# The head of an attention, MoE and FFN kernel: w loaded as rows and turned, u loaded as one row and spread by a product with ones

## The chip, the cores and the metric

The kernel runs on one core of a Trainium2 chip. The metric is device time in microseconds of one execution; lower is better. Inputs and the output are float32 in DRAM.

## What is computed

Three stages follow each other. The first is a linear attention with decay, for 4 batches, 8 heads, 768 steps and head size 48; `w` (8 x 48) is the decay per head and channel, `u` (8 x 48) a factor for the current step:

```python
for t in range(S):
    kt, vt, rt = (k[:, :, t], v[:, :, t], r[:, :, t])
    cur = np.einsum('bhd,bhe->bhde', u[None] * kt, vt)
    y[:, :, t] = np.einsum('bhd,bhde->bhe', rt, state + cur)
    state = w[None, :, :, None] * state + np.einsum('bhd,bhe->bhde', kt, vt)
```

Its output, 3072 rows of 384, goes through a soft mixture of 8 experts (`phi`, `w1`, `w2`), and then through a feed-forward layer of width 2048 with an ELU (`w_in`, `w_out`).

## The kernel before

The attention works in 6 chunks of 128 steps; a unit is one chunk of one batch (24 units, `UNITS`). Inside a unit the decay is taken out by tables of powers of w: r is multiplied by w to the power of the step (`tables_T[:, 0]`), k by its inverse (`tables_T[:, 1]`), so that scores are one product of turned r and turned k. Heads stand in pairs, 64 partitions for each, of which 48 are used (`HP`, `D`). The five engines each run their own program, written out by hand, and meet in semaphores.

The head, up to the first scores, goes as follows.

- **SyncE** (`sync`) waits for GpSimd's first memset (`cleared`), loads w twice into `wcol`, transposed by the access pattern (`w_cols`, L428 to L431), one copy for each half of the partitions, then the first r (`load_r(0, 0)`, three DMAs from `load`, L375 to L377). Then it waits for the first k and loads k, r and v of batches 2 and 3, two pieces of w1, and goes on to the loop `load_chunk`, which refills k, r and v of each pair of batches when their readers are done.
- **ScalarE** (`scalar`) loads the first k (L375 to L377), does one Exp (L1292) that brings its table in, loads u into `u_row`, the same row for all 128 partitions (L1293), copies w into `wpow` (L1296, `w_copied`), issues four loads of phi (L1301), waits for the doubled table and copies its swapped half (L1304, `table_swapped`), loads the first v, and copies the turned table out of PSUM to `k_table` (L1307).
- **GpSimd** (`gpsimd`) sets constants (L488 to L519), waits for u and k, and forms r*u*k of units 0 and 1 in four products (L544, L547, twice); later it scales k (L527) and forms the same products for the following units (L535, L538).
- **VectorE** (`vector`) waits for w (`w_loaded`), takes its reciprocal (L996), and doubles the tables in six steps of two products (L1004 squares the powers, L1007 doubles the table), then L1014 twice, L1019 (which waits for `table_swapped`) and L1022. After it come r into `r_pair` (L1035), k into `k_pair` (L1080), the sum of r*u*k (`bonus`, L1028), k of unit 1 scaled into `k_nat` (L1084), and r and bonus of unit 1.
- **TensorE** (`tensor`) starts when `ones` is set with four products of ones (L598) whose results nobody reads, of 512, 512, 256 and 256 columns, then turns r of unit 0 (L603), k (L626), r of unit 1, and the table (L739); `keep_clock_up` (L593) adds products of ones; `attend` (L643) makes the scores. `turn_k(1, ...)` waits for L1084 (`k_scaled`), and then `key_values` (L667) needs the first v.

The loop after that repeats per unit: `key_values`, turns, state, values, scores. The expert and feed-forward stages follow; the diff does not touch them.

## Time and profile before

| | us |
|---|---|
| median of 3 runs | 393.62 |
| lowest and highest | 391.74, 393.88 |
| profiled execution | 392.18 |
| its span, first to last instruction | 390.4 |
| TensorE busy | 374.2 |
| VectorE, ScalarE, GpSimd busy | 267.6, 219.6, 103.3 |

The page gives busy time of each engine, then the span in 40 slices of 9.8 us (a digit is a tenth of a slice), then the chain that ended last. A timeline row gives the start, the duration, the engine, the line and what is written from what, and in brackets how long the engine stood idle before it and what ended that. ACTq and SPq rows are DMA issues: their duration is the issuing, not the transfer.

### The profile page before, as it was taken

The numbers are of one execution on the slowest core, as the hardware profiler recorded it, in microseconds if no ns is written. First come the engines' busy times: TensorE is split into PE (matmuls) and PEld (weight loads), VectorE is DVE, ScalarE is ACT, GpSimd is POOL, SyncE is SP. The second block draws the span as 40 slices with busy tenths as digits, with TensorE's granted clock in tenths as the row PEclk, the third lists the DMA queues.
The fourth block names the chain that finished last, engine by engine and source line by source line (L and its number), as shares of the span: only waits on it lengthen the run. The fifth ranks groups of instructions, "written<-read, shape, count | busy, mean of one in ns | idle before, by whom it ended". The sixth has DMA issues, their size and how long they took to land.

```text
span 390.4 us, 11439 instructions
## 1 busy us (share of the span) xinstructions
PE 374.2 (96%) x4373; PEld 333.0 (85%) x4373; DVE 267.6 (69%) x512; ACT 219.6 (56%) x498; POOL 103.3 (26%) x136
## 2 busy tenths in 40 slices
PE   6898999999889999999999999999999999999996
PEld 3787898989775454589999999999999999999996
DVE  4787788778767620699867767667777667776671
ACT  2896778777772131588564446444644464455441
POOL 7797777777640000355200000000000000000000
PEclk9999999999999999999999999999999999999999
DMA  7989899999999999920020002000200020002002
GB/s 152 254 151 186 199 234 233 227 255 254 235 303 426 430 432 403 373 64 2 0 83 1 2 0 81 0 0 0 81 0 0 0 81 0 0 0 82 2 2 81
DMA packets 87280, 51.80 MB, mean 133 GB/s; under 512 B 77776, under 2 KB 83024, under 8 KB 85200
## 3 DMA queue, kind: packets, MB, share of 16 engines
q1 hardware_dynamic: 82368, 50.21, 43.1%
q10 hardware_dynamic: 4880, 1.16, 1.4%
q8 instruction: 19, 0.31, 0.3%
q14 instruction: 13, 0.11, 0.1%
HBM read 45.86 MB, written 4.72 MB: 130 GB/s over the span
## 4 chain that ended last, share of the span: by engine, by line
PE 79%; DMA 10%; SPq 3%; issue 3%; ACT 3%; DVE 1%; POOL 1%; DVEq 0%; POOLq 0%; ACTq 0%
PE psum L976 17%; PE psum L978 17%; PE psum L977 17%; PE psum L911 6%; DMA w_out_raw<-in_moe_w_out_dram 4%; PE psum L603 4%; DMA r_raw<-in_r_dram 3%; PE psum L643 3%; PE psum L826 3%; PE psum L686 3%; PE psum L667 2%; PE psum L656 2%; PE psum L696 2%; DMA v_sb<-in_v_dram 1%; PE psum L703 1%
## 5 line engine op out<-in xcount | busy, mean ns | idle before, releaser
L978 PE MATMUL psum<-w_out_hi,elu_lo 128*128 128x384 f32 x372 | 125.8, 338 | 0.0
L976 PE MATMUL psum<-w_out_hi,elu_hi 128*128 128x384 f32 x372 | 125.7, 338 | 0.0
L977 PE MATMUL psum<-w_out_lo,elu_hi 128*128 128x384 f32 x372 | 125.3, 337 | 0.0
L1405 ACT ACTIVATE exp_h<-psum 128x512 f32<-128x512 f32 x96 | 57.6, 600 | 97.3 <-PE psum L911 97.0
L1246 DVE SCALAR_TENSOR_TENSOR elu<-psum,neg_part 128x512 f32<-128x512 f32 x96 | 66.3, 690 | 57.1 <-ACT neg_part L1392 57.1
L977 PEld LDWEIGHTS psum<-w_out_lo,elu_hi 128*128 128x128 f32 x372 | 69.8, 188 | 3.9
L976 PEld LDWEIGHTS psum<-w_out_hi,elu_hi 128*128 128x128 f32 x372 | 70.4, 189 | 0.0
L978 PEld LDWEIGHTS psum<-w_out_hi,elu_lo 128*128 128x128 f32 x372 | 69.9, 188 | 0.0
L1238 DVE TENSOR_TENSOR elu_lo<-elu,elu_hi 128x512 fp32r<-128x512 f32 x96 | 66.3, 691 | 0.6
L1280 ACT ACTIVATE scores<-ident_wide,bonus 128x128 f32<-128x128 f32 x192 | 58.8, 390 | 5.0 <-DVE bonus L1028 4.9
L1392 ACT ACTIVATE neg_part<-exp_h 128x512 f32<-128x512 f32 x96 | 60.0, 626 | 1.7 <-DVE elu L1246 1.3
L1259 DVE CAST elu_hi<-elu 128x512 fp32r<-128x512 f32 x96 | 44.0, 458 | 0.6
L1041 DVE COPY_PREDICATED scores<-mask,psum 128x512 f32<-128x512 uint32 x48 | 33.3, 736 | 15.3 <-PE psum L643 12.9
L911 PE MATMUL psum<-c_T,G_T 128*128 (+1 forms) x96 | 37.6, 397 | 0.8 <-DMA G_T<-G_parts 0.6
L686 PE MATMUL psum<-scores,v_sb 64*64 64x128 f32 (+1 forms) x768 | 25.9, 245 | 1.8 <-issue 1.6
L527 POOL TENSOR_TENSOR k_nat<-k_raw,k_table 128x384 f32<-128x384 f32 x23 | 23.2, 1009 | 15.6 <-PE psum L667 7.9
L584 POOL TENSOR_TENSOR w_out_lo<-w_out_raw,w_out_hi 128x384 fp32r<-128x384 f32 x16 | 16.8, 1058 | 34.4 <-ACT w_out_hi L1387 34.4
L686 PEld LDWEIGHTS psum<-scores,v_sb 64*64 64x64 f32 x768 | 22.4, 133 | 2.8 <-issue 2.8
L538 POOL TENSOR_TENSOR k_raw<-k_raw,r_raw 128x384 f32<-128x384 f32 x22 | 22.1, 1006 | 6.0 <-DMA r_raw<-in_r_dram 4.7
L643 PE MATMUL psum<-r_pair,k_pair 48*64 48x128 f32 (+1 forms) x768 | 20.9, 245 | 1.8 <-DVE r_pair L1035 1.8
L535 POOL TENSOR_TENSOR k_raw<-k_raw,u_row 128x384 f32<-128x384 f32 x22 | 22.1, 1006 | 1.7
L911 PEld LDWEIGHTS psum<-c_T,G_T 128*128 128x128 f32 x96 | 18.1, 190 | 3.5 <-issue 1.7
(155 smaller groups left out, 403.6 us busy)
## 6 DMA issues: line engine op xcount, KB each, us to landing
w<-in_moe_w_dram SPq DMA_DIRECT2D x8, 1536.0 KB, 13.6
w_sb<-in_moe_w_dram SPq DMA_DIRECT2D x8, 1024.0 KB, 6.3
out_dram<-out_sb SPq DMA_DIRECT2D x24, 192.0 KB, 1.9
w_sb<-in_moe_w_dram SPq DMA_DIRECT2D x8, 512.0 KB, 6.2
w_out_raw<-in_moe_w_out_dram SPq DMA_DIRECT2D x4, 768.0 KB, 15.7
r_raw<-in_r_dram SPq DMA_DIRECT2D x12, 192.0 KB, 3.2
r_raw<-in_r_dram SPq DMA_DIRECT2D x24, 96.0 KB, 3.4
w_in_sb<-in_moe_w_in_dram SPq DMA_DIRECT2D x1, 2304.0 KB, 19.4
```

The costliest lines, as they stand in the source:

```text
L686: m = pe.matmul(ps_y[e * HP:e * HP + HP, two, q * P + cols.start:q * P + P], v_sb[rows, q, b, 2 * e + two, :], scores[rows, i, h, cols], s ...
L911: pe.matmul(banks[4 + f % RING][:, :], G_T[:, f * P:(f + 1) * P], c_T[:, bass.ds(i * BANK, BANK)], start=True, stop=True).then_inc(ffn_don ...
L976: pe.matmul(acc, hi, w_out_hi[:, f, :], start=(f == 0), stop=False)
L977: pe.matmul(acc, hi, w_out_lo[:, f, :], start=False, stop=False)
L978: m = pe.matmul(acc, lo, w_out_hi[:, f, :], start=False, stop=(f == KF2 - 1))
L1041: dve.copy_predicated(scores[:, i, two::2, :].rearrange("p (n a) t -> p n a t", n=2), mask[:, :, :].bitcast(U32).unsqueeze(2).broadcast_to ...
L1238: dve.tensor_tensor(elu_lo[:, f % RING, :], elu[:, f % 2, :], elu_hi[:, f % RING, :].bitcast(F32), ALU.subtract).then_inc(lo_done, 1)
L1246: dve.scalar_tensor_tensor(out=elu[:, f % 2, :], in0=banks[4 + f % RING][:, :], scalar=0.0, in1=neg_part[:, f % 2, :], op0=ALU.max, op1=AL ...
L1259: dve.tensor_copy(elu_hi[:, f % RING, :], elu[:, f % 2, :]).then_inc(hi_done, 1)
L1280: m = act.activation(scores[:, i, h, :], ident if h < H // 2 else ident_swap, ACT.Copy, scale=bonus[:, i, h:h + 1])
L1392: act.activation(neg_part[:, f % 2, :], exp_h[:, f % 2, :], ACT.Relu, bias=1.0, scale=-1.0).then_inc(neg_ready, 1)
L1405: act.activation(exp_h[:, f % 2, :], banks[4 + f % RING][:, :], ACT.Exp).then_inc(exp_done, 1)
```

## The change

- w is loaded once, as 8 rows of twice 48 numbers, into a corner of `tables_T` (`w_nat`) that GpSimd fills with ones before. TensorE turns it twice, into two PSUM banks (`ps_w`); VectorE reads its reciprocals from one, ScalarE copies its powers from the other. Both now wait for `w_turned`.
- u is loaded as one row into partition 0 of `u_row`, by ScalarE ahead of k. TensorE multiplies it with a column of ones into PSUM (`u_spread`), and ScalarE copies the result over `u_row` (`u_ready`), for which GpSimd now waits. The table is turned into the bank of the second copy of w only after `w_copied` and `u_ready`.
- The first v is issued by SyncE right behind the first r, no longer by ScalarE.
- Two of the four products of ones stand ahead of the new turns, two behind.

```diff
--- before.py
+++ after.py
@@ -115,7 +115,6 @@
         state_sum = place("state_sum", [P, PAIRS, D], F32)
         bonus = place("bonus", [P, 2, H], F32)
         mask = place("mask", [P, 2, P], F32)
-        wcol = place("wcol", [P, H], F32)
         wpow = place("wpow", [P, 8, 2, PAIRS], F32)
         exp_warm = place("exp_warm", [P, 1], F32)
         ATT_END = cursor[0]
@@ -213,6 +212,9 @@
         ps_x = banks[7].rearrange("p (a t) -> p a t", a=PAIRS)
         ps_k_first = psum[:, 2:4, 0:PAIRS * HP].rearrange("p s (a t) -> p s a t", a=PAIRS)
         ps_tab = banks[4].rearrange("p (h d) -> p h d", h=H)
+
+        w_nat, u_nat = tables_T[0:H, 0, 0, :], u_row[0:1, :, :].rearrange("p h d -> p (h d)")
+        ps_w, ps_u = (banks[4][:, 0:H], banks[0][:, 0:H]), banks[1][:, 0:DM]
         ps_warm = banks[5][:, 0:P]
 
 
@@ -230,7 +232,10 @@
         v_loaded = [sem(f"v_loaded{g}") for g in range(2)]
         u_loaded = sem("u_loaded")
         w_loaded = sem("w_loaded")
+        w_turned = sem("w_turned")
         w_copied = sem("w_copied")
+        u_spread = sem("u_spread")
+        u_ready = sem("u_ready")
         phi_loaded = sem("phi_loaded")
         w1_loaded = sem("w1_loaded")
         w2_loaded = [sem(f"w2_loaded{e}") for e in range(E)]
@@ -327,7 +332,6 @@
             return x.rearrange("b (i rev) t d -> rev b t i d", rev=2)
 
         r_dram, k_dram, v_dram = by_sets(r), by_sets(k), by_sets(v)
-        w_cols = w.rearrange("h d -> d h")
         u_flat = u.rearrange("h d -> (h d)").rearrange("(o n) -> o n", o=1)
         phi_rows = phi.rearrange("(half two q d) s -> half two d q s", q=2, half=2, two=2)
         w1_dram = w1.rearrange("e (p c) f -> e p c f", p=P)
@@ -381,9 +385,10 @@
             return x_sb[:, UNITS - 2 + un, 0:DM].rearrange("p (rev i d) -> p rev i d", rev=2, d=D)
 
 
-        w_halves = [(slice(two * HP, two * HP + HP),
-                     wcol[two * HP:two * HP + HP, :].rearrange("p (e two rev) -> p two rev e", two=2, rev=2)[:, two])
-                    for two in range(2)]
+        w_halves, w_halves_too = (
+            [(slice(two * HP, two * HP + HP),
+              turned[two * HP:two * HP + HP, :].rearrange("p (e two rev) -> p two rev e", two=2, rev=2)[:, two])
+             for two in range(2)] for turned in ps_w)
 
         block = ctx.enter_context(nc.Block())
 
@@ -426,10 +431,9 @@
                         load_w1(range(2, E), slice(2, KD))
 
             sp.wait_ge(cleared, 1)
-            for half in range(2):
-                sp.dma_start(wcol[half * HP:half * HP + D, :], w_cols, allow_slow_non_contiguous=True
-                             ).then_inc(w_loaded, 16)
+            sp.dma_start(w_nat.rearrange("h (two d) -> h two d", two=2)[:, :, 0:D], w.unsqueeze(1).broadcast_to([H, 2, D])).then_inc(w_loaded, 16)
             load_r(0, 0)
+            load_v(0, 0)
             sp.wait_ge(k_loaded[0], LOADED)
             load_k(0, 1)
             load_r(0, 1)
@@ -485,7 +489,7 @@
 
         @block.gpsimd
         def _(pool):
-            pool.memset(wcol[:, :], 1.0).then_inc(cleared, 1)
+            pool.memset(w_nat, 1.0).then_inc(cleared, 1)
             pool.memset(v_sb[:, :, :, :, D:HP], 0.0).then_inc(cleared, 1)
             pool.memset(phi_sb[:, :, :], 0.0).then_inc(cleared, 1)
             pool.memset(ones[:, :], 1.0).then_inc(ones_set, 1)
@@ -538,7 +542,7 @@
                 pool.tensor_tensor(k_raw[:, :, b], k_raw[:, :, b], r_raw[:, :, b, :, 0:D], ALU.mult).then_inc(ruk_done, 1)
 
 
-            pool.wait_ge(u_loaded, 16)
+            pool.wait_ge(u_ready, 1)
             pool.wait_ge(k_loaded[0], LOADED)
             for un in range(2):
                 pool.tensor_tensor(ruk_first(un), k_raw[:, :, un], u_sets, ALU.mult).then_inc(ru_done, 1)
@@ -594,9 +598,21 @@
 
 
             pe.wait_ge(ones_set, 1)
-            for i, n in ((2, 4), (3, 4), (6, 2), (5, 2)):
+            def fill(i, n):
                 pe.matmul(banks[i][:, 0:n * P].rearrange("p (n t) -> p n t", n=n), ones[:, :],
                           ones[:, :].unsqueeze(1).broadcast_to([P, n, P]), start=True, stop=True)
+
+            fill(2, 4)
+            fill(6, 2)
+
+            pe.wait_ge(const_set, 5)
+            pe.wait_ge(w_loaded, 16)
+            for at in ps_w:
+                pe.transpose(at, w_nat, ident[0:H, 0:H]).then_inc(w_turned, 1)
+            pe.wait_ge(u_loaded, 16)
+            pe.matmul(ps_u, ones[0:1, :], u_nat, start=True, stop=True).then_inc(u_spread, 1)
+            fill(3, 4)
+            fill(5, 2)
 
             def turn(turned, nat, last_pairs):
                 for a in range(PAIRS):
@@ -728,13 +744,14 @@
                 return m
 
 
-            pe.wait_ge(const_set, 5)
+            pe.wait_ge(w_copied, 1)
             pe.wait_ge(pads_set, 1)
             turn_r(0, 0, 0)
             pe.wait_ge(k_loaded[0], LOADED)
             turn_k_first()
             turn(banks[7], r_pair_raw(1), ident_swap).then_inc(r_turned, 1)
             pe.wait_ge(tables_done, 3)
+            pe.wait_ge(u_ready, 1)
             for a in range(PAIRS):
                 m = pe.transpose(banks[4][:, a * P:(a + 1) * P], tables_T[:, 1, a, :], ident[:, :])
             m.then_inc(table_turned, 1)
@@ -990,7 +1007,7 @@
 
 
 
-            dve.wait_ge(w_loaded, 32)
+            dve.wait_ge(w_turned, 2)
             dve.memset(tables_T[:, 0, :, HP:HP + 1], 1.0).then_inc(powers, 1)
             for rows, cols in w_halves:
                 m = dve.reciprocal(wpow[rows, 0, 1, :].rearrange("p (rev e) -> p rev e", rev=2), cols)
@@ -1287,14 +1304,16 @@
                          ps_y[:, :, 0:2 * P].rearrange("p two (q t) -> p two q t", q=2)).then_inc(yT_ready, 1)
 
 
+            act.dma_start(u_nat, u_flat).then_inc(u_loaded, 16)
             load(act, k_raw, k_dram, 0, 0, k_loaded)
             act.wait_ge(const_set, 5)
             act.activation(exp_warm[:, :], ident[:, 0:1], ACT.Exp)
-            act.dma_start(u_row[:, :, :].rearrange("p h d -> p (h d)"), u_flat.broadcast_to([P, DM])).then_inc(u_loaded, 16)
-            act.wait_ge(w_loaded, 32)
-            for rows, cols in w_halves:
+            act.wait_ge(w_turned, 2)
+            for rows, cols in w_halves_too:
                 m = act.copy(wpow[rows, 0, 0, :].rearrange("p (rev e) -> p rev e", rev=2), cols)
             m.then_inc(w_copied, 1)
+            act.wait_ge(u_spread, 1)
+            act.copy(u_row[:, :, :].rearrange("p h d -> p (h d)"), ps_u).then_inc(u_ready, 1)
             act.wait_ge(cleared, 3)
             for half in range(2):
                 for two in range(2):
@@ -1302,7 +1321,6 @@
                                   ).then_inc(phi_loaded, 16)
             act.wait_ge(powers, 15)
             act.copy(tables_T[:, 1, 2:PAIRS, 0:HP], tables_T[:, 1, 2:PAIRS, HP:P]).then_inc(table_swapped, 1)
-            load(act, v_sb, v_dram, 0, 0, v_loaded)
             act.wait_ge(table_turned, 1)
             act.copy(k_table[:, :, :], ps_tab[:, :, 0:D]).then_inc(table_ready, 1)
             diagonals(0, 0, 0)
```

TensorE at the start of its program, before (names: `ident_wide` is the identity; L598 are the products of ones, L603 turns, L626 turns of k, L739 the turned table):

```order
L598 MATMUL psum<-ones 128x512 [waits ones_set]
L598 MATMUL psum<-ones 128x512
L598 MATMUL psum<-ones 128x256 x2
L603 MATMUL psum<-ident_wide,r_raw 128x128 [waits r_loaded0,pads_set,const_set]
L603 MATMUL psum<-ident_wide,r_raw 128x128 x3
L626 MATMUL psum<-ident_wide,k_raw 48x64 [waits k_loaded0]
L626 MATMUL psum<-ident_wide,k_raw 48x64 x15
L603 MATMUL psum<-ident_wide,r_raw 128x128 x4
L739 MATMUL psum<-ident_wide,tables_T 128x128 [waits tables_done]
L739 MATMUL psum<-ident_wide,tables_T 128x128 x3
```

and in the changed kernel (L602 products of ones, L611 the turns of w, L613 the product for u, L619 turns, L642 turns of k, L756 the turned table):

```order
L602 MATMUL psum<-ones 128x512 [waits ones_set]
L602 MATMUL psum<-ones 128x256
L611 MATMUL psum<-ident_wide,tables_T 128x8 [waits w_loaded,const_set]
L611 MATMUL psum<-ident_wide,tables_T 128x8
L613 MATMUL psum<-u_row,ones 128x384 [waits u_loaded]
L602 MATMUL psum<-ones 128x512
L602 MATMUL psum<-ones 128x256
L619 MATMUL psum<-ident_wide,r_raw 128x128 [waits r_loaded0,pads_set,w_copied]
L619 MATMUL psum<-ident_wide,r_raw 128x128 x3
L642 MATMUL psum<-ident_wide,k_raw 48x64 [waits k_loaded0]
L642 MATMUL psum<-ident_wide,k_raw 48x64 x15
L619 MATMUL psum<-ident_wide,r_raw 128x128 x4
L756 MATMUL psum<-ident_wide,tables_T 128x128 [waits u_ready,tables_done]
L756 MATMUL psum<-ident_wide,tables_T 128x128 x3
```

Between the products of ones now stand three products that wait for the loads of w and u, and the table's turn waits for `u_ready` besides.

ScalarE from its table load to the copy of the turned table, before:

```order
L1292 ACTIVATE exp_warm<-ident_wide 128x1 [waits const_set]
L1293 DMA u_row<-in_u_dram 128x384
L1296 COPY wpow<-wcol 64x4 [waits w_loaded]
L1296 COPY wpow<-wcol 64x4
L1301 DMA phi_sb<-in_moe_phi_dram 48x2x32 [waits cleared]
L1301 DMA phi_sb<-in_moe_phi_dram 48x2x32 x3
L1304 COPY tables_T<-tables_T 128x2x64 [waits powers]
L375 DMA v_sb<-in_v_dram 128x8x48
L376 DMA v_sb<-in_v_dram 64x8x48
L377 DMA v_sb<-in_v_dram 64x8x48
L1307 COPY k_table<-psum 128x384 [waits table_turned]
```

and in the changed kernel, where the issue of u (L1307) stands ahead of the three of k:

```order
L1310 ACTIVATE exp_warm<-ident_wide 128x1 [waits const_set]
L1313 COPY wpow<-psum 64x4 [waits w_turned]
L1313 COPY wpow<-psum 64x4
L1316 COPY u_row<-psum 128x384 [waits u_spread]
L1320 DMA phi_sb<-in_moe_phi_dram 48x2x32 [waits cleared]
L1320 DMA phi_sb<-in_moe_phi_dram 48x2x32 x3
L1323 COPY tables_T<-tables_T 128x2x64 [waits powers]
L1325 COPY k_table<-psum 128x384 [waits table_turned]
```

The issues of phi (`phi_sb`) stand behind the copy of u out of PSUM, the copy inside `tables_T` comes behind them as before, and the three issues of v are gone.

## Rows read from the trace of the kernel before

**Rows 1.** The page: busy time of TensorE, and the DMA share in 40 slices.
```profile
PE 374.2 (96%) x4373; PEld 333.0 (85%) x4373; DVE 267.6 (69%) x512; ACT 219.6 (56%) x498; POOL 103.3 (26%) x136
...
DMA  7989899999999999920020002000200020002002
```

**Rows 2.** The chain of waits, head (start us, us, what).
```profile
3.34 4.47 DMA r_raw<-in_r_dram
...
12.20 0.63 PE psum L603 x4
...
13.94 0.52 PE psum L667 x16
...
14.62 1.00 POOL k_nat L527
```

**Rows 3.** Timeline, ScalarE (start, us, engine, line, op, out<-in, [idle before <-releaser]).
```profile
0.82 0.47 ACTq L375 DMA_DIRECT2D k_raw<-in_k_dram  x1
...
4.49 0.20 ACT L1296 COPY wpow<-wcol 64x4 f32<-64x4 f32 x1 [0.21 <-DMA wcol<-in_w_dram]
...
4.87 1.42 ACTq L1301 DMA_DIRECT2D phi_sb<-in_moe_phi_dram  x3
6.78 0.30 ACT L1304 COPY tables_T<-tables_T 128x128 f32<-128x128 f32 x1 [1.89 <-DVE tables_T L1007]
6.79 0.43 ACTq L375 DMA_DIRECT2D v_sb<-in_v_dram  x1
...
10.23 0.48 ACT L1307 COPY k_table<-psum 128x384 f32<-128x384 f32 x1 [3.15 <-PE psum L739]
```

**Rows 4.** Timeline, VectorE.
```profile
6.32 0.43 DVE L1007 TENSOR_TENSOR tables_T<-tables_T,wpow 128x256 f32<-128x256 f32 x1
...
7.33 0.28 DVE L1019 TENSOR_TENSOR tables_T<-tables_T,wpow 128x128 f32<-128x128 f32 x1
...
8.68 0.69 DVE L1035 TENSOR_TENSOR r_pair<-psum,tables_T 128x512 f32<-128x512 f32 x1 [1.00 <-PE psum L603]
...
10.74 1.36 DVE L1084 TENSOR_TENSOR k_nat<-k_raw,k_table 128x384 f32<-128x384 f32 x1 [0.28 <-ACT k_table L1307]
```

**Rows 5.** Timeline, GpSimd.
```profile
7.55 1.00 POOL L544 TENSOR_TENSOR x_sb<-k_raw,u_row 128x384 f32<-128x384 f32 x1 [1.46 <-DMA u_row<-in_u_dram]
...
10.67 1.01 POOL L547 TENSOR_TENSOR x_sb<-x_sb,r_raw 128x384 f32<-128x384 f32 x1
```

**Rows 6.** Timeline, GpSimd and VectorE in chunk 1.
```profile
31.47 1.01 POOL L538 TENSOR_TENSOR k_raw<-k_raw,r_raw 128x384 f32<-128x384 f32 x1 [0.17 <-DMA r_raw<-in_r_dram]
31.54 1.01 DVE L1057 COPY logits_T<-logits_now 128x128 f32<-128x128 f32 x1
```

**Rows 7.** Timeline, TensorE, head (PEld is a weight load).
```profile
1.72 4.50 PE L598 MATMUL psum<-ones 128*128 128x512 f32 x8 [1.72 <-POOL ones L491]
2.74 0.34 PEld L598 LDWEIGHTS psum<-ones 128*128 128x128 f32 x1 [0.52 <-issue]
...
3.59 0.34 PEld L598 LDWEIGHTS psum<-ones 128*128 128x128 f32 x1 [0.52 <-issue]
...
5.19 0.62 PEld L598 LDWEIGHTS psum<-ones 128*128 128x128 f32 x3 [0.41 <-issue]
...
7.95 0.63 PE L603 MATMUL psum<-ident_wide,r_raw 128*128 128x128 f32 x4 [1.73 <-DMA r_raw<-in_r_dram]
```

**Rows 8.** Stretch 4 to 6 us (last: clock, DMA share, GB/s); v loads; SyncE issues.
```profile
4.00:6.00 2.00, 2.00 (x6) 0.91 (x4) 1.45 (x14) 0.66 (x4) 1.53 (x7) 1.00 1.23 262
...
DMA to landing us min/median/max: 3.3/4.1/5.3
...
6.12 0.39 SPq L375 DMA_DIRECT2D k_raw<-in_k_dram  x1
...
14.82 0.38 SPq L375 DMA_DIRECT2D k_raw<-in_k_dram  x1
...
17.17 2.90 SPq L375 DMA_DIRECT2D r_raw<-in_r_dram  x1
```

## The prediction

> **What bounds the kernel now.** I read the page first: TensorE is busy 96% of the span and the DMA engines are near full for the first half [rows 1]. The diff touches only the head, so what counts is when TensorE gets into its steady row of work, and whether a later stage passes a shift on. The chain of waits shows the head [rows 2]: the last piece of the first r lands 4.47 us after 3.34, at 7.81; TensorE turns r at 7.95 [rows 7], needs the scaled k of unit 1 at 12.20 and multiplies k and v from 13.94; GpSimd scales the k of unit 2 at 14.62. From there on the chain is TensorE, with waits on loads that consumers release. I take 14.6 us as the hand-over point: what the change has won or lost there I carry to the end.
>
> The profiled execution took 392.18 us around its span of 390.4; the median of the three runs is 393.62, which is 1.4 higher. My shift is worked out in the profiled execution and added to the median.
>
> **Loads.** w was 2 DMAs with a packet for every number, now one of 16 rows; SyncE saves one issue of about 0.5, so r is issued from 1.4 instead of 2.02. u was 192 KB (one row to 128 partitions), now 1.5 KB; its issue, some 0.45, now stands ahead of k's, which moves from 0.82 to 1.3 [rows 3]. Both feed the same engines, which move 262 GB/s in the stretch from 4 to 6 us [rows 8]: k and r are 768 KB, 2.9 us of that rate. Starting near 2.5 they are in by about 6.0 to 6.3. k was in at 6.1 (SyncE, which waits for it, goes on at 6.12) [rows 8], so k gains nothing, r about 1.6. The first v (3 issues) goes into SyncE's gap from 3.96 to 6.12, where they fit; it used to leave ScalarE at 6.79 to 8.80 [rows 3] and land 3.3 to 5.3 after issue [rows 8], by some 13.4, under TensorE's warm-up products that end at 13.94. I cost that move at nothing; without that cover its gain would count.
>
> **TensorE's head.** A warm-up product of 512 columns is two passes of 0.85 (2.74 to 3.59); from 5.19 on three weight loads, one per pass of 256 columns, take 0.62 together, so a pass is some 0.2, half the time per column [rows 7]. So the clock was at 1.2 GHz until about 5.1 and at 2.4 after it, with unbroken work from 1.72 on. (The granted clock is printed as 1.00 in the stretch from 4 to 6 us, so the steps tell more here than that column.) Now fills of 512 and 256 columns end at 1.72 + 1.71 + 0.85 = 4.28. The two turns of w: four warm turns of 128 columns take 0.63 [rows 7], so at most 0.3 each at half clock and at least a bare load and 8 columns, 0.15: w is turned at 4.6 to 4.9; I take 4.8. The product for u, 384 columns in two passes, is 0.64 at 2.4 GHz and 1.28 at 1.2 (from the same steps); begun cold and ended warm it is done at about 5.65. ScalarE copies 128x384 out of PSUM in 0.48 [rows 3]: u is ready at 6.2, instead of 7.5. Fills of 512 and 256 columns follow, 1.28 warm: 5.6 to 6.95. So r is turned from 6.95, 1.0 earlier than 7.95; the fills, not r, end last.
>
> **ScalarE.** The table load and exp ended at 4.28 (0.21 idle before 4.49); they move 0.5 later, still about when w is turned. But the four phi issues, 1.8 us (0.34 + 1.42 and gaps), used to start at 4.50 and now stand behind the copy of u: 6.2 to 8.0. Queued behind them is the copy that swaps the table (0.30, formerly 6.78) [rows 3]. VectorE's last table step waits for it, so its next step, r into r_pair, cannot start before 8.0 + 0.30 + 0.28 + 0.15 + gaps = 8.8; it was 8.68 [rows 4]. Thus r_pair gains nothing at all even though r comes 1.6 earlier. The turned table does gain, since TensorE reaches it sooner: at 8.7 to 9.35. ScalarE copied it to k_table from 10.23 to 10.71; now it can at 9.4 to 9.9 [rows 3].
>
> **VectorE against GpSimd, the term that decides.** GpSimd was free at 6.09 and waited 1.46 for u before its four products of 1.0 each [rows 5]. They began at 7.55, when the table chain was practically over (7.61). Now k and u are there at 6.2, so the four products start near 6.3, while VectorE, 0.4 later than before (4.8 plus the copies of w), still has 1.4 us of table products ahead. What happens then is seen once in this head: L1084, a product of two SBUF operands, 128x384, started at 10.74 beside GpSimd's L547 (10.67 to 11.68) and took 1.36 [rows 4, 5]. By the 128 and 256 column products (0.28, 0.43) it should take 0.57; it ended 0.42 after GpSimd's product did. The copy L1057 at 31.54 took 1.01 beside L538, and ended with it too [rows 6]. So a VectorE instruction of this kind stands until GpSimd's is over. In the Trainium skill, SBUF — State Buffer, Who interferes with whom, says that a VectorE instruction with two SBUF inputs contends with a GpSimd instruction that reads SBUF, and that whoever issued second blocks fully. By that rule the sum comes to +0.2 to +1.3 (below), and to the first rival's -0.95 without it; L1084 agrees.
>
> All remaining table products are of that kind, and they hang on each other. Bounds: one block (GpSimd takes the first turn and VectorE's row then runs through) puts r_pair at about 9.15; four blocks in turn put it at about 11.0. I take two, the middle of what the gaps between dependent products allow: VectorE stands from 6.4 to 7.3, works to 8.05, stands to 9.05, and the last table step ends near 9.9. Then r_pair 9.95 (was 8.68), k_pair until 11.3, the reduction (0.54) until 11.85, k_nat (0.57) until 12.45, instead of 12.10. Sum at 12.2: r and the turned table earlier, but **+0.35 us** net (one block +0.2, since k_nat then meets GpSimd's fourth product; four blocks k_nat ends at 13.4, +1.3; and -0.1 if k_nat finds GpSimd idle).
>
> **Does the shift last?** The copy of k_nat is followed by the turn, five fills and key_values, as before. SyncE's issues are slowed by full queues (the r load at 17.17 took 2.90) [rows 8]. With 190 KB and some 770 tiny packets gone its row runs about 1 us ahead, so no load becomes the new end. Later loads are released by consumers, the weights of the experts too, so they shift along. 393.62 + 0.35 is about **393.9 us**. A difference under 0.5%, 2.0 us, is about what a measurement of this kernel cannot tell from none.
>
> **Rivals.**
> 1. *No block, or one that fits in.* If the products run side by side, r_pair is at 8.8, k_pair ends at 10.2, the reduction at 10.65, and k_nat, alone, at 11.15: -0.95, so 392.7. For it: the table step at 7.33 still ran when GpSimd began at 7.55 and took its 0.28 [rows 4, 5], though there VectorE was first. Against it: L1084. Chance 0.25.
> 2. *The clock stays low.* TensorE's unbroken row is cut at 4.3 by the tiny turns and the wait for u. If it stays at 1.2 GHz past 5.1, the u product takes 1.28 and the fills 2.56, r is turned at 8.8 (+0.85). If it stays there until 12.2, the turns and products between 7.95 and 10.2 (2.25 us) take twice that, less what VectorE's lateness hides: up to +1.9 more, 2.7 in all, 396.3. This is the slower side; it passes 0.5% only if the clock is still low through most of the turns up to about 11 us. For it: before, the clock rose after an unbroken row. Against: once up it stayed up through the idle 1.73 ahead of 7.95 [rows 7]: the four turns behind it took 0.63. Chance 0.13.
> 3. *The load stream was the bound.* If the attention stage runs on SyncE's row, what counts is when k of the next chunk is issued: 14.82 before [rows 8], at best 12.9 with unslowed issues; -1.9, 391.7. Against: TensorE waits for loads only briefly before 36 us. Chance 0.12.
> 4. The forecast, two blocks or its neighbours: 0.50.
>
> **Numbers.** From 391.7 (rival 3) to 396.0 (the clock for most of the head) and the spread of 2 us between runs: 391.5 to 396.0. Faster by over 0.5%: most of rival 3 and a little of rival 1, 0.13. Slower: rival 2's upper part and four blocks that grow later, 0.15. Between: 0.72.
>
> **What would show it.** In the changed profile: GpSimd's first product near 6.3; a table product of about 1 us beside it; r_pair's first step after 9; k_nat's end at 12.3 to 13.4; weight loads of 0.19 from about 5.2 on. The steps are wrong if all table products keep their 0.16 to 0.43 (rival 1), if the fills before r show 0.34 weight loads (rival 2), or if the span falls by more than what is won at 14.6 us (rival 3). If u is ready after 7.5, the collision term falls.

## The result, and the profile after

| | before | changed |
|---|---|---|
| median of 20 runs each, us | 393.71 | 394.82 |
| lowest and highest | 391.56, 395.65 | 391.8, 398.3 |
| ratio, 95% interval | | 1.0054 [1.0032, 1.0076] |
| profiled execution, its span | 392.18, 390.4 | 394.29, 392.6 |

The ratio leaves out two executions of the changed kernel, 398.14 and 398.3, that lie over 1.5% above its fastest. By it the change costs 0.5%, about 2.1 us, just over the bound up to which the prediction spoke of no change; the two medians of the table differ by less, 1.11 us or 0.28%. So the cost is clear of zero, but its size is known only as 0.3% to 0.8%. The forecast of 393.9 is 0.9 below the measured median. What was forecast as +0.35 us at the end of the head came out as +2.0 there.

The page of the changed kernel, lines of its parts 1 and 4:

```profile
PE 377.5 (96%) x4377; PEld 334.4 (85%) x4377; DVE 269.2 (69%) x512; ACT 220.5 (56%) x499; POOL 104.6 (27%) x136
...
PE 81%; DVE 5%; DMA 4%; issue 3%; SPq 3%; ACT 1%; POOL 1%; POOLq 0%; DVEq 0%
```

TensorE has 3.3 us more [rows 1]: a share of that is the product for u and products of ones at half clock. VectorE, which held 1% of the chain before and nothing of its first 17 us, holds 5% of it, 18.9 us, of which 8.5 lie in the first 17 us. The rest lies behind the head, and the split differs between single executions (16.7 and 3.7 in the second profile). The chain of waits of the changed kernel, head (start, us, what):

```profile
7.43 0.87 DVE wpow L1021
...
8.67 1.51 DVE tables_T L1031 x2
...
10.91 0.95 DVE wpow L1039
...
11.89 0.69 DVE r_pair L1052
```

Before, the chain up to 12.20 was the load of r and TensorE's turns [rows 2]; now it is the table of powers on VectorE. The timeline shows why. GpSimd and VectorE (L1021, L1024, L1031 and L1039 are table products, as L1036 is, L548 and L551 GpSimd's products of r, u and k, L521 and L523 GpSimd's memsets; a VectorE row's start can lie a little before the end of the one ahead of it):

```profile
5.10 0.17 DVE L1013 RECIPROCAL wpow<-psum 64x4 f32<-64x4 f32 x1 [5.10 <-issue]
5.36 0.31 POOL L521 MEMSET k_nat<- 128x256 f32 x1
5.50 0.69 DVE L1016 COPY tables_T<-wpow 128x4 f32<-128x4 f32 x1
...
5.86 0.31 POOL L523 MEMSET state<- 128x256 f32 x1
6.23 0.17 DVE L1024 TENSOR_TENSOR tables_T<-tables_T,wpow 128x8 f32<-128x8 f32 x1
...
7.01 0.16 DVE L1021 TENSOR_TENSOR wpow<-wpow 128x8 f32<-128x8 f32 x1
7.13 1.15 POOL L548 TENSOR_TENSOR x_sb<-k_raw,u_row 128x384 f32<-128x384 f32 x1 [0.97 <-ACT u_row L1316]
7.34 0.96 DVE L1021 TENSOR_TENSOR wpow<-wpow 128x8 f32<-128x8 f32 x1
8.36 1.14 POOL L551 TENSOR_TENSOR x_sb<-x_sb,r_raw 128x384 f32<-128x384 f32 x1
8.67 2.12 DVE L1031 TENSOR_TENSOR tables_T<-tables_T,wpow 128x256 f32<-128x256 f32 x2
9.46 1.18 POOL L548 TENSOR_TENSOR x_sb<-k_raw,u_row 128x384 f32<-128x384 f32 x1
...
10.71 1.13 POOL L551 TENSOR_TENSOR x_sb<-x_sb,r_raw 128x384 f32<-128x384 f32 x1
10.91 0.95 DVE L1039 TENSOR_TENSOR wpow<-wpow 128x4 f32<-128x4 f32 x1
...
13.56 0.55 DVE L1101 TENSOR_TENSOR k_nat<-k_raw,k_table 128x384 f32<-128x384 f32 x1
```

Each of GpSimd's four products has one VectorE product that stands until it is over: L1021 ends at 8.30 and GpSimd's first at 8.28; L1039 ends at 11.86 and the fourth at 11.84. L1021 works on 8 columns and took 0.16 when nothing stood beside it, as at 7.01. The groups by shape (busy us, mean ns) part the two L1031, the second and third block, and L1039:

```profile
L1031 DVE TENSOR_TENSOR tables_T<-tables_T,wpow 128x256 f32<-128x256 f32 x1 | 1.1, 1107 | 0.0
L1031 DVE TENSOR_TENSOR tables_T<-tables_T,wpow 128x128 f32<-128x128 f32 x1 | 1.1, 1085 | 0.0
L1039 DVE TENSOR_TENSOR wpow<-wpow 128x4 f32<-128x4 f32 x1 | 1.0, 954 | 0.0
```

GpSimd pays too: 1.13 to 1.18 us a product where it took 1.00 [rows 5].

SyncE, ScalarE and TensorE of the changed kernel in the same stretch:

```profile
6.58 0.38 SPq L379 DMA_DIRECT2D k_raw<-in_k_dram  x1
...
6.57 0.48 ACT L1316 COPY u_row<-psum 128x384 f32<-128x384 f32 x1 [1.16 <-PE psum L613]
6.58 2.46 ACTq L1320 DMA_DIRECT2D phi_sb<-in_moe_phi_dram  x4
9.08 0.30 ACT L1323 COPY tables_T<-tables_T 128x128 f32<-128x128 f32 x1 [2.04 <-DVE tables_T L1024]
...
4.91 1.62 PE L613 MATMUL psum<-u_row,ones 1*128 1x384 f32 x2
6.46 2.93 PE L602 MATMUL psum<-ones 128*128 128x512 f32 x4
7.48 0.34 PEld L602 LDWEIGHTS psum<-ones 128*128 128x128 f32 x1 [0.52 <-issue]
9.19 0.94 PE L619 MATMUL psum<-ident_wide,r_raw 128*128 128x128 f32 x4
```

k is in at 6.57 (SyncE goes on at 6.58; 6.12 before [rows 8]). The product for u ends at 6.53 and the fills (the products of ones) start at 6.46 with weight loads of 0.34, the step of half clock [rows 7]. r is turned from 9.19 instead of 7.95.

**The sum, now from measured rows.** The reciprocals start 0.60 later (5.10; 4.50 before). The copy L1016, 0.69 for an operation that takes 0.17 elsewhere, puts the chain back by another 0.54: the first doubling L1024 starts at 6.23, and at 5.09 before, so 1.14 in all. The four blocks cost 0.80 + 0.68 + 0.80 + 0.80 = 3.08. From the old end of the table, 7.68, that gives 11.90, and the row ends at 11.86. VectorE used to stand idle 1.00 there [rows 4], so r_pair starts 3.21 later (11.89). Of this 1.19 comes back by k_nat: with GpSimd finished, k_nat takes 0.55 instead of 1.36, there is no wait of 0.28 for k_table, and the rest is 0.10 of gaps. k_nat ends at 14.11 instead of 12.09: **+2.02 us**.

### The profile page after: what moved, and what is told of

The parts are those of the page before. It is cut to its first block, busy times and chain, and to the rows that moved or that the text cites. A ratio compares the mean times of both kernels' runs of the same rounds, so it can differ in the third digit from the quotient of the medians.

```text
span 392.6 us, 11449 instructions
## 1 busy us (share of the span) xinstructions
PE 377.5 (96%) x4377; PEld 334.4 (85%) x4377; DVE 269.2 (69%) x512; ACT 220.5 (56%) x499; POOL 104.6 (27%) x136
## 4 chain that ended last, share of the span: by engine, by line
PE 81%; DVE 5%; DMA 4%; issue 3%; SPq 3%; ACT 1%; POOL 1%; POOLq 0%; DVEq 0%
PE psum L993 17%; PE psum L994 17%; PE psum L995 17%; PE psum L928 6%; DMA r_raw<-in_r_dram 4%; PE psum L619 3%; PE psum L659 3%; PE psum L702 3%; PE psum L863 3%; PE psum L843 3%; PE psum L712 2%; PE psum L672 2%; PE psum L683 2%; SPq L380 1%; SPq L379 1%
## 5 line engine op out<-in xcount | busy, mean ns | idle before, releaser
L659 PEld LDWEIGHTS psum<-r_pair,k_pair 48*64 48x64 f32 x768 | 18.9, 133 | 4.9 <-issue 4.6
```

The lines of the kernel that those rows point to most:

```text
L659: m = pe.matmul(ps_A[two][e0:e0 + HP, a, cols], k_pair[rows, i, a, e0:e0 + HP], r_pair[rows, i, a, cols], start=True, stop=True, skip_grou ...
```

## Experiments

All runs compute the whole of the reference; none leaves a part out. Each was compared with the kernel before in runs on the same chip. Three chips were used, so kernels are set against each other by their ratios and not by their medians. "k_nat" is the end of its first product, the head's last step: 12.09 before, 14.11 changed. Times of steps come from the one profiled execution of each kernel.

### GpSimd's products wait for the table

```diff
             pool.wait_ge(u_ready, 1)
+            pool.wait_ge(tables_done, 3)
+            pool.wait_ge(powers, DECAY_SET)
             pool.wait_ge(k_loaded[0], LOADED)
```

> The changed kernel, but GpSimd starts its four products of k, u and r only when VectorE's table chain is through (tables_done 3 and the last power). Theory A (the collision of these products with the table products is the main loss): table products keep 0.16 to 0.43 us, r_pair starts near 10.2 instead of 11.89 (then TensorE's late turn of r ends last), k_nat ends near 13.2 instead of 14.11, and the first scores start 1 us or more earlier than 13.29; the time falls by about 1 us against the changed kernel. Theory B (the low clock of TensorE is the main loss): r_pair at 10.2 too, but k_nat and the first scores move by less than 0.4 us, time unchanged within 0.3 us.

Measured: 394.48 of 12 runs, ratio 1.0014 [0.9979, 1.0049]. The rows that the collision had stretched:

```profile
7.36 0.16 DVE L1023 TENSOR_TENSOR wpow<-wpow 128x8 f32<-128x8 f32 x1
...
7.94 0.63 DVE L1033 TENSOR_TENSOR tables_T<-tables_T,wpow 128x256 f32<-128x256 f32 x2
9.43 0.29 DVE L1038 TENSOR_TENSOR tables_T<-tables_T,wpow 128x128 f32<-128x128 f32 x1 [0.86 <-ACT tables_T L1325]
9.64 0.15 DVE L1041 TENSOR_TENSOR wpow<-wpow 128x4 f32<-128x4 f32 x1
10.04 1.00 POOL L550 TENSOR_TENSOR x_sb<-k_raw,u_row 128x384 f32<-128x384 f32 x1 [3.85 <-DVE wpow L1041]
10.36 0.69 DVE L1054 TENSOR_TENSOR r_pair<-psum,tables_T 128x512 f32<-128x512 f32 x1 [0.56 <-PE psum L621]
12.67 0.82 DVE L1103 TENSOR_TENSOR k_nat<-k_raw,k_table 128x384 f32<-128x384 f32 x1
```

With the four products away, every table product has its own duration again, and the table is ready at 9.79 instead of 11.86. So the blocks are shown: the same instructions, less only what stood beside them. The first scores start at 12.50 (13.29 changed), 0.8 earlier where the expectation wanted 1 or more. The time moved from 1.0054 to 1.0014, but the two intervals overlap, so the gain is seen in the head and not shown in the time. And k_nat gains just 0.62 (13.49), because two things that the blocks had covered now show: the swap stands behind the phi issues (0.86 idle), and r's turn ends last (0.56 idle); and the delayed GpSimd products meet the reduction and k_nat instead.

### The product for u behind all products of ones; and both edits together

```diff
-            pe.wait_ge(u_loaded, 16)
-            pe.matmul(ps_u, ones[0:1, :], u_nat, start=True, stop=True).then_inc(u_spread, 1)
             fill(3, 4)
             fill(5, 2)
+            pe.wait_ge(u_loaded, 16)
+            pe.matmul(ps_u, ones[0:1, :], u_nat, start=True, stop=True).then_inc(u_spread, 1)
```

> The changed kernel, but TensorE's product for u stands behind all four products of ones, so only the two tiny turns of w interrupt them. Theory A: the clock does not matter much; the collision stays (u is ready near 7.5, the products start near 7.6 and still meet three table products), k_nat ends at 13.5 or later. Theory B: the record of the clock starts at 5 to 6 us instead of 9.86, r is turned from about 7.3, and k_nat ends 1 us or more earlier. If the clock record still starts after 8 us, the two turns of w alone are enough to hold the clock low.

> Both edits together: products of GpSimd behind the table chain, product for u behind the products of ones. If A and B each hold a part, r_pair starts near 9.6 (bound by phi issues and the swapped copy on ScalarE), k_nat ends near 12.3 as in the kernel before, and the time is within 0.3% of the kernel before. If neither is the cause, the time stays at 1.005 of before.

Measured: alone 397.43 of 11 runs, 1.0083 [1.005, 1.0116]; with GpSimd's wait 395.73 of 12, 1.0054 [1.0023, 1.0084]. The first is the slowest kernel of the study. ScalarE of the first of them:

```profile
8.82 0.48 ACT L1316 COPY u_row<-psum 128x384 f32<-128x384 f32 x1 [3.40 <-PE psum L615]
8.83 1.92 ACTq L1320 DMA_DIRECT2D phi_sb<-in_moe_phi_dram  x4
10.79 0.30 ACT L1323 COPY tables_T<-tables_T 128x128 f32<-128x128 f32 x1 [1.49 <-issue]
```

Of the first expectation only "k_nat ends at 13.5 or later" came true (14.73), with u ready at 9.30 and not at 7.5; the second wanted k_nat near 12.3 and the time within 0.3% of before, and neither came. The clock did rise earlier, at 7.94 and 7.17 by the trace's record (9.86 changed), and r was turned from 8.71 and 8.38 (9.19). The copy of u waits 3.40, the four phi issues wait behind it in ScalarE's program, and the swap behind those; the table ends at 12.48 and, in the combination, at 11.14. In the first one whole block is left (L1039, 0.96 from 11.53) and a short one (L1036, 0.48), in the second none, and the queue on ScalarE has taken their place. In the combination k_nat ends latest of all (14.83), since the reduction waits for GpSimd products that begin at 11.38. So these two runs show what a late u costs on ScalarE; they don't weigh the blocks against the clock.

### v issued by SyncE, alone

```diff
             load_r(0, 0)
+            load_v(0, 0)
...
-            load(act, v_sb, v_dram, 0, 0, v_loaded)
```

> The kernel before with the one edit that SyncE issues the first v right behind the first r. The prediction costed it at nothing: first scores at 10.6 us, key_values at 13.9, ratio to before within 0.998 to 1.002. Rival: v ahead in the queue delays k (it stood between k, w and r) and the loads of batches 2 and 3, so the first k lands after 6.5, GpSimd is unaffected (it waits for u till 7.5), and the time rises by 0.3 to 1 us.

Measured (kernel before with this move): 394.65 of 12 runs, 1.0007 [0.9974, 1.0041]; k_nat 12.26, +0.17, which is what the kernel before shows in its own second profile (12.27). Costed at nothing in the prediction, and it is nothing that these runs can tell.

### The two halves of the change

The changed kernel with u loaded to 128 partitions as before (w and v changed):

```diff
-            pool.wait_ge(u_ready, 1)
+            pool.wait_ge(u_loaded, 16)
...
-            pe.wait_ge(u_loaded, 16)
-            pe.matmul(ps_u, ones[0:1, :], u_nat, start=True, stop=True).then_inc(u_spread, 1)
...
-            pe.wait_ge(u_ready, 1)
...
-            act.dma_start(u_nat, u_flat).then_inc(u_loaded, 16)
...
+            act.dma_start(u_row[:, :, :].rearrange("p h d -> p (h d)"), u_flat.broadcast_to([P, DM])).then_inc(u_loaded, 16)
...
-            act.wait_ge(u_spread, 1)
-            act.copy(u_row[:, :, :].rearrange("p h d -> p (h d)"), ps_u).then_inc(u_ready, 1)
```

> The changed kernel with u loaded as before (one DMA of 192 KB to 128 partitions, issued by ScalarE behind its Exp) and no product for u. Theory A (collision): u lands at about 7.5 as before, so GpSimd's products start near 7.6 while the table chain, which starts at 5.1, ends near 8.4 undisturbed: two or three table products still meet them, r_pair near 10 to 10.5, k_nat's end at 12.8 to 13.4. Rival (the early start of the table chain's own inputs matters, not GpSimd): the table chain starts at 5.1, 0.6 after before, and k_nat's end is 0.6 late, 12.7, with no table product over 0.6 us except the copy of the reciprocal (0.7, beside memsets).

And the kernel before with the u part alone (the same lines the other way round, the product between the fills of 512 and 256 and of 512 and 256 columns):

> The kernel before with only u changed: one row, product with ones, copy out of PSUM, GpSimd waits for that. Theory A: the table chain starts at 4.5 and would end at 7.6; u is ready near 6.8, k near 6.3, so GpSimd starts near 6.9 and meets two table products; the phi issues stand behind the copy of u and end near 8.9, so the swapped copy comes at 8.9 instead of 6.8; r_pair near 9.6 to 10.5, k_nat's end 12.8 to 13.3. Rival: u earlier is harmless or good, r_pair at 8.7 to 9.0, k_nat's end at 12.1 or before.

Measured: w and v 394.01 of 12, 1.0020 [0.9981, 1.0058], k_nat 12.87, +0.78; u alone 393.55 of 12, 1.0026 [0.9991, 1.0061], k_nat 13.22, +1.13. The shifts add up to 1.91 against 2.02 for the whole, the ratios to 0.46% against 0.54%. Neither half alone can be told from no change in time. Both halves collide:

w and v, where u lands by its own load and only the table is late (two blocks; the second is on L1036, 0.96 from 9.48):

```profile
7.92 1.43 DVE L1028 TENSOR_TENSOR tables_T<-tables_T,wpow 128x256 f32<-128x256 f32 x2
8.19 1.02 POOL L548 TENSOR_TENSOR x_sb<-k_raw,u_row 128x384 f32<-128x384 f32 x1 [2.01 <-DMA u_row<-in_u_dram]
```

u alone, where GpSimd starts 0.66 earlier, and the table's first doubling waits 0.39 for ScalarE's copy of w (three blocks):

```profile
6.89 0.99 POOL L547 TENSOR_TENSOR x_sb<-k_raw,u_row 128x384 f32<-128x384 f32 x1 [0.79 <-ACT u_row L1305]
7.02 2.14 DVE L1020 TENSOR_TENSOR tables_T<-tables_T,wpow 128x256 f32<-128x256 f32 x2
8.88 1.06 PE L609 MATMUL psum<-ident_wide,r_raw 128*128 128x128 f32 x4
9.09 1.08 DVE L1025 TENSOR_TENSOR tables_T<-tables_T,wpow 128x128 f32<-128x128 f32 x1
```

### Also the swap ahead of the phi issues

```diff
+            act.wait_ge(powers, 15)
+            act.copy(tables_T[:, 1, 2:PAIRS, 0:HP], tables_T[:, 1, 2:PAIRS, HP:P]).then_inc(table_swapped, 1)
             act.wait_ge(cleared, 3)
...
-            act.wait_ge(powers, 15)
-            act.copy(tables_T[:, 1, 2:PAIRS, 0:HP], tables_T[:, 1, 2:PAIRS, HP:P]).then_inc(table_swapped, 1)
```

This, and GpSimd's wait of the first experiment.

> The changed kernel, GpSimd's products behind the table chain as in e1_products_wait, and ScalarE's four phi issues behind the copy that swaps the table. If the phi issues were the next limit: the last table product ends near 8.7 instead of 9.79, GpSimd starts near 8.9 instead of 10.04, and k_nat's end comes 0.6 to 1.0 before the 13.49 of e1. If TensorE's late turn of r (9.2 with the clock low) is the limit instead, r_pair stays at 10.2 to 10.4 and only GpSimd moves, k_nat's end within 0.4 of 13.49.

Measured: 394.41 of 12, 1.0051 [1.0013, 1.0089]. The table is done at 8.82, 3.0 earlier than in the changed kernel, and r_pair still starts at 10.36:

```profile
9.19 1.06 PE L621 MATMUL psum<-ident_wide,r_raw 128*128 128x128 f32 x4
10.36 0.69 DVE L1054 TENSOR_TENSOR r_pair<-psum,tables_T 128x512 f32<-128x512 f32 x1 [1.54 <-PE psum L621]
12.55 1.05 DVE L1103 TENSOR_TENSOR k_nat<-k_raw,k_table 128x384 f32<-128x384 f32 x1 [0.27 <-ACT k_table L1327]
```

VectorE now idles 1.54 for r's turn, which the fills at half clock hold until 9.19. k_nat ends at 13.60, no better than 13.49. k_nat itself takes 1.05 instead of 0.55, beside GpSimd's fourth product. The second bound under the blocks is TensorE.

### Rearranged: w turned once, one product of ones fewer, no collision

```diff
-            fill(6, 2)
...
-            for at in ps_w:
+            for at in ps_w[:1]:
                 pe.transpose(at, w_nat, ident[0:H, 0:H]).then_inc(w_turned, 1)
...
-            fill(5, 2)
+            fill(6, 2)
...
-            dve.wait_ge(w_turned, 2)
+            dve.wait_ge(w_turned, 1)
+            for rows, cols in w_halves:
+                m = dve.tensor_copy(wpow[rows, 0, 0, :].rearrange("p (rev e) -> p rev e", rev=2), cols)
+            m.then_inc(w_copied, 1)
...
+                if un == 1:
+                    pool.wait_ge(k_scaled, 1)
```

Besides these, the two edits of the last experiment; GpSimd's fourth product now waits for k_nat (`k_scaled`), and ScalarE's copies of w are gone.

> A try for a version that beats both: w is turned once, behind the first product of ones (near 3.6), VectorE copies w itself, one product of ones of 256 columns less, swapped copy ahead of the phi issues, GpSimd's products behind the table chain and its last one behind k_nat. The table chain starts near 4.1 and ends near 7.5; r lands at 7.2, is turned from 7.3 to 8.0; r_pair near 8.4, k_nat alone near 10.7 to 11.3 (12.09 before); the ratio to before 0.997 to 1.000. If it is not below 1.000 although k_nat's end is early, the head's gain is lost behind it (k of unit 0 scaled by GpSimd).

Measured: 393.01 of 12 runs, 1.0004 [0.9972, 1.0035]; k_nat 12.49. w is turned behind one fill only, the copy into the table starts before GpSimd's memsets and takes 0.17, the table ends at 7.86, and r_pair waits 1.54 for r's turn until 9.39. The time can't be told from that of before.

### w so, and u as before

```diff
             load_r(0, 0)
-            load_v(0, 0)
...
-            pool.wait_ge(u_ready, 1)
+            pool.wait_ge(u_loaded, 16)
...
+            load(act, v_sb, v_dram, 0, 0, v_loaded)
```

The w part as in the last kernel, with all four products of ones, three of them behind the turn of w; u (its load by ScalarE to all 128 partitions) and v as before; GpSimd's products no longer wait for the table, only the fourth waits, for k_nat.

> A second try for a version that beats both: the kernel before with w as rows, turned once behind the first product of ones and copied by VectorE; u and v loaded as before; GpSimd's last product behind k_nat. Table chain from near 4.2 to near 7.4, GpSimd from 7.5 (u's landing) so it meets nothing, clock up by 5 to 8 us, r turned at 7.7 to 8.0, k_nat undisturbed and ended at 11.1 to 11.4 (12.09 before). Ratio to before 0.997 to 1.000, which five rounds can hardly tell from 1.

Measured: 394.73 of 13 runs, 1.0025 [0.9987, 1.0063]. In the head it is the best kernel of all: k_nat ends at 10.92, 1.17 earlier than before, as k_nat stands beside no GpSimd product and takes 0.55. That GpSimd would meet nothing did not hold: its first product starts at 7.45, and L1037, a table product of 128 columns, takes 1.09 beside it instead of 0.28. The time doesn't show the gain. The rows show where it goes in this one execution (it took 401.88, 7 above the median, and the trace's clock drops at 47 and at 122 us, so its later part is not read):

```profile
7.51 1.09 DVE L1037 TENSOR_TENSOR tables_T<-tables_T,wpow 128x128 f32<-128x128 f32 x1
...
13.35 0.56 PE L682 MATMUL psum<-v_sb,k_nat 128*48 128x48 f32 x16 [0.58 <-DMA v_sb<-in_v_dram]
...
19.70 0.43 PE L701 MATMUL psum<-scores,v_sb 64*64 64x128 f32 x8 [1.60 <-issue]
```

The first v, again issued late by ScalarE, is what key_values waits for; half of the gain is gone there (13.35, and 13.87 before), and an idle stretch of 1.60 on TensorE for which no releaser is shown takes the rest. Whether v moved to SyncE would keep the gain wasn't tried, and with one execution profiled, and an unusually long one, it stays open whether the idle stretch belongs to the kernel: where the gain goes in the others is not shown.

### The product for u first of all

```diff
-            fill(2, 4)
...
+            pe.wait_ge(u_loaded, 16)
+            pe.matmul(ps_u, ones[0:1, :], u_nat, start=True, stop=True).then_inc(u_spread, 1)
             pe.wait_ge(const_set, 5)
             pe.wait_ge(w_loaded, 16)
...
-            pe.wait_ge(u_loaded, 16)
-            pe.matmul(ps_u, ones[0:1, :], u_nat, start=True, stop=True).then_inc(u_spread, 1)
+            fill(2, 4)
             fill(3, 4)
             fill(6, 2)
```

The rearranged kernel with nothing ahead of the product for u and the turn of w.

> As e8_rearranged, but TensorE's product for u is its first instruction, w's turn the second, and the products of ones follow without a break. Clock theory (a product of one row, 1.6 us at the low clock, inside the row of products of ones delays the clock): the record of the full clock starts at 6 to 8 us instead of 10.37, r is turned near 7.7 and k_nat ends near 11.7 instead of 12.49. Rival (the record's start is chance, 5 to 11 us in any kernel): it starts anywhere, also after 9.

Measured: 392.64 of 12 runs, 0.9987 [0.9948, 1.0025]. It loads w, u and v as the change does, and its interval lies below that of the changed kernel (whose lower end is 1.0032), though the two were not run against each other; from before it can't be told. VectorE and TensorE:

```profile
4.83 0.17 DVE L1021 COPY tables_T<-wpow 128x4 f32<-128x4 f32 x1
...
3.80 4.63 PE L606 MATMUL psum<-ones 128*128 128x512 f32 x6
8.22 1.06 PE L621 MATMUL psum<-ident_wide,r_raw 128*128 128x128 f32 x4
9.39 0.69 DVE L1057 TENSOR_TENSOR r_pair<-psum,tables_T 128x512 f32<-128x512 f32 x1 [1.73 <-PE psum L621]
```

The table is done at 7.66, and k_nat ends at 12.10, as before the change. What failed is the expectation on the clock: the row of fills from 3.80 on is unbroken and all at half clock (each pass of 512 columns 0.85 as in [rows 7]), and r's turn takes 1.06 instead of 0.63; VectorE idles 1.73 for it.

### Each kernel once more

> The changed kernel once more, for a second profile. The collision theory expects at least three table instructions of 0.9 us or more again and r_pair after 11; the clock theory expects the full clock from after 9 us again (9.86 in the first profile). If either is chance, it differs here.

> The kernel before once more, for a second profile. No table instruction over 0.5 us, GpSimd's first product at 7.5 to 7.7, r_pair at 8.7 to 9.0, k_nat's end near 12.1; full clock from 5 to 8 us (5.08 in the first profile, 7.53 in e4_v_by_sync_alone whose TensorE row is the same).

Measured: changed 395.02, span 393.3; before 393.35, span 391.6. Of the changed kernel the blocked rows return to within 0.02 us:

```profile
7.33 0.96 DVE L1021 TENSOR_TENSOR wpow<-wpow 128x8 f32<-128x8 f32 x1
8.66 2.12 DVE L1031 TENSOR_TENSOR tables_T<-tables_T,wpow 128x256 f32<-128x256 f32 x2
```

k_nat ends at 14.10; in the second look at before, at 12.27. What did move in before is the clock: the trace's record of its full level starts at 5.08 in the first look and at 7.47 in the second.

### All runs on one line

If a shift of the head went through to the end undiminished, a ratio should be the shift of k_nat over 393.7:

| kernel | k_nat ends | shift | as a ratio | measured, interval |
|---|---|---|---|---|
| u first, rearranged | 12.10 | +0.01 | 1.0000 | 0.9987 [0.9948, 1.0025] |
| v by SyncE alone | 12.26 | +0.17 | 1.0004 | 1.0007 [0.9974, 1.0041] |
| rearranged | 12.49 | +0.40 | 1.0010 | 1.0004 [0.9972, 1.0035] |
| w and v | 12.87 | +0.78 | 1.0020 | 1.0020 [0.9981, 1.0058] |
| u alone | 13.22 | +1.13 | 1.0029 | 1.0026 [0.9991, 1.0061] |
| products wait | 13.49 | +1.40 | 1.0036 | 1.0014 [0.9979, 1.0049] |
| and swap first | 13.60 | +1.51 | 1.0038 | 1.0051 [1.0013, 1.0089] |
| changed | 14.11 | +2.02 | 1.0051 | 1.0054 [1.0032, 1.0076] |
| u product last | 14.73 | +2.64 | 1.0067 | 1.0083 [1.005, 1.0116] |
| both | 14.83 | +2.74 | 1.0070 | 1.0054 [1.0023, 1.0084] |
| w early, u as before | 10.92 | -1.17 | 0.9970 | 1.0025 [0.9987, 1.0063] |

All but the last lie in their intervals, and the four kernels with the largest shifts, the changed one among them, are the four whose intervals lie wholly above 1. So a shift to the later side fits with passing on in full. More is not shown: the intervals are about as wide as the shifts, seven of the eleven hold 1.0000 as well, and the kernel before differs by 0.18 in k_nat's end between its own two profiles. The one clear gain did not show in the time.

## Why the prediction was right, and where it was not

- **The number.** The measured 394.82 lies between 391.5 and 396.0, and by the ratio the change is just over the 0.5% that parted "between" (0.72) from "slower" (0.15). That it lies in the range is in part luck: at the end of the head the prediction allowed its own mechanism +0.2 to +1.3, and +2.02 came. The upper end of the range was set for another reason, a clock low through most of the head (whose own worst case was 396.3).
- **The collision.** The mechanism, VectorE's table products standing behind GpSimd's, is shown by the first experiment. What was mis-sized is "I take two": four blocks came, in turn with GpSimd's four products. The section Who interferes with whom of SBUF — State Buffer in the Trainium skill says that the instruction issued second blocks fully; this trace agrees, with L1021 held for 0.96 where it takes 0.16, and ended 0.02 after GpSimd's. GpSimd's products are slowed as well, by 0.13 to 0.18. Because the table products hang on each other, one is always waiting when GpSimd's product ends, and GpSimd's next one is issued while VectorE's runs.
- **Even the four-block bound was short.** It said 13.4 for k_nat's end and 11.0 for r_pair; they were 14.11 and 11.89. Missing were 0.54 for the copy L1016 beside the memsets, which no sentence of the prediction had, and w turned later than "4.6 to 4.9": the first fills did not end at 4.28, the turns only start at 4.68 and are read at 5.10. GpSimd began at 7.13 and not near 6.3: u's product, two passes of 0.8 at half clock and so 1.62 where even the low-clock price was 1.28, ended at 6.53, and the copy out of PSUM at 7.05; k had come at 6.57. It began later, and still found four products of the table ahead of it, because the table was later as well.
- **The loads.** "r about 1.6" was 0.6: its last piece landed at 7.22 and at 7.81 before, and not at 6.0 to 6.3. It cost nothing in the changed kernel, where the fills hold TensorE until 9.19.
- **phi behind u.** "6.2 to 8.0" was 6.58 to 9.04: four issues of 2.46 in all, where before they took 0.34 + 1.42. In the changed kernel the blocks hide it; the products-wait kernel shows it as 0.86 idle.
- **TensorE's head, and rival 2.** "r is turned from 6.95" was 9.19, and the rise of the clock at 5.1 did not come: the fills still load weights in 0.34. The rival was right about the clock and had a chance of 0.13; it said 8.8, where its own terms, 4.8 + 1.28 + 2.56, give 8.64. It did not set the time: r_pair waited for the table until 11.89, while r's turn was done at about 10.1. It is the next bound, and in the kernels without the blocks it is the one that is seen (1.54 and 1.73 idle).
- **Rival 1**, no block, fell: its -0.95 needed table products of 0.16 to 0.43 beside GpSimd. **Rival 3**, the load stream, fell too: SyncE reached its w1 issue earlier (12.38, and 13.60 before), but the next k, which its readers release, went out at 15.32 and not 14.82 [rows 8], and the scores came 2.0 later. That issues are slowed "by full queues" is an inference; the rows show only how long they take.
- **The shift lasts.** Right as far as these runs can tell. Scores of the third and fourth unit are 2.0 later; the last of 24 starts 1.0 later in the one profile and 1.6 in the second (against their own look at before), the expert stage 3.2 and 2.9, the span 2.2 and 1.7 longer. The kernel before alone differs by 1.1 at the expert stage between its two profiles. In between single executions differ by idle stretches of TensorE without a shown releaser (1.48 at 114.83 and 1.00 at 121.77 in the changed kernel), so the table above over many runs is the better evidence.

## What to carry to other kernels

When a load is made faster, look at what its reader does once it is released: here GpSimd's four products were free as long as they came after the table, and cost 3.1 us of the table's chain when released into it. Of a chain of small dependent VectorE products like this one, count a block for every GpSimd product that can be issued beside it (four of four here, three with u alone, two with w and v), and keep the two apart by order. And before removing a bound, write down the next two under it: here ScalarE's issues and TensorE's clock stood right behind the blocks, so that taking the blocks away gave back 0.6 of 2.0 us.

## What the runs showed of the hardware that was not expected

**A copy beside memsets.** L1016 copies 4 columns and took 0.69 in the changed kernel, from 5.50 to 6.19, beside three memsets of GpSimd, the last of which ends at 6.17; it took 0.17 where it stood ahead of them (4.83 in the u-first kernel). L1021, issued behind it at 5.59, ends with it. Table products of up to 32 columns took 0.16 to 0.19 beside the same memsets in the kernel before, as they do elsewhere, so it is the copy and not any VectorE instruction. That the memsets hold it is read from these ends and not tested by moving them.

**A row of ones and the clock.** Start of the full clock (2.4 GHz; the lower level is 1.2) in the trace's record, by where the product of one row stands on TensorE (in one kernel, w and v, no usable value; there weight loads are down to 0.19 from 5.54 on):

| product of one row (K = 1) | starts of full clock, us |
|---|---|
| none in the head: before twice, v by SyncE, w early | 5.08, 7.47, 7.53, 6.23 |
| behind all fills: alone, and with GpSimd's wait | 7.94, 7.17 |
| ahead of or within the fills: changed twice, products wait, u alone, swap first, rearranged, u first | 9.86, 9.34, 10.77, 11.19, 10.53, 10.37, 9.47 |

In these 13 profiles the first two groups and the third do not overlap. The gap between them is 1.4 us (7.94 to 9.34). The pause before the second fills isn't it: in the u-first kernel the fills run unbroken from 3.80 and the clock still comes at 9.47. But wherever the product of one row comes early, the row of fills that nothing larger than the turns of w interrupts also starts later, at 3.80 to 6.47 instead of 1.72 or 1.82, and no run has the one without the other. So it is not shown that the product of one row, 384 columns in two passes, is what puts the clock off. The same instructions differ from run to run as well (5.08 and 7.47 in before), and in before that moved k_nat's end by only 0.18.

**GpSimd beside VectorE** is slowed as well: each of its four products took 1.13 to 1.18 us where it took 1.00 before. Holding a VectorE product up is not by itself what slows it: before, the fourth held L1084 and took 1.01 [rows 4, 5], and with w and v L548 held L1028 and took 1.02. What does is open.
